# One fused kernel (attention, routed experts, gated convolution): an earlier load of the third pair, and another way through the routing

## The chip, the cores and the metric

The kernel runs on one core of a Trainium2 chip. A core has five engines that run at the same time and wait for each other by semaphores: TensorE (PE, matrix products and transposes), VectorE (DVE), ScalarE (ACT), GpSimd (POOL) and SyncE (SP, which issues transfers). The metric is the device time of one execution in microseconds (us); lower is better.

## The reference, cut to what matters

```python
# attention, per batch (4) and head (8), S = 576 positions, 64 wide
cum = cumsum(max(s, 0)); bias = min(-(cum_i - cum_j), 0)
attn = softmax(causal(q @ k.T / 8 + bias)); x = attn @ v          # x: [4, 576, 512]
# mixture: each token goes to one expert of E = 8
for s in range(S):
    fresh_e = argmax(logits[b, s])
    e = fresh_e if s == 0 or local_gate[b, s] < 0.5 else prev_e   # keeps the last token's expert
    out[b, s] = p[e] * (relu(x[b, s] @ w1[e]) @ w2[e])
# third part: relu(x @ w_in), a convolution of 3 taps along S, sigmoid gate, @ w_out
```

A token whose local gate is 0.5 or more takes the expert of the token before it, so the expert of each token depends on all tokens before it in its batch.

## The kernel before, in words

**Attention** goes over 16 pairs of heads. Each pair's q, k and v come in as natural rows, TensorE turns them (q_nat and k_nat to q_tr and k_tr), and scores are made in nine units per pair. GpSimd makes a bias tile for each unit from ncum_row and ncum_tail, which SyncE loads for each pair from a DRAM copy of the running sums. VectorE adds it to the score (L511), ScalarE takes the exponential, TensorE turns the probabilities (L310) and multiplies with v (L407, L417). The order on each engine is written out by hand; q, k, v and the sums have two buffers each. TensorE multiplies each pair's result with an identity beside the gate weights (L368), so that x and the pair's share of the gate logits come out together; VectorE scales both by the row sums (scale_gates, normalise, and their _end forms for the last tiles). add_heads (L599) sums the eight heads' shares after the last pair of a batch.

**SyncE's queue** is one list (L158 to L191): the sums and q of pair 0, k of pair 1 and sums for pairs 0 and 1; then v of pairs 0 and 1, the gate weights (sync_early, L876 to L880), and then for each pair p: q and k of p + 2, a piece of the first experts' weights, v and sums.

**Routing** follows the last pair. vector_route finds each token's best expert and a code (rank_code: 8 minus its number, or 0 where the token keeps the last expert). Tokens lie in 20 tiles, 5 for each of 4 batches, the fifth with 64 tokens. TensorE turns the codes into 4 rows of 576, one for each batch (L932); VectorE carries the last code that isn't 0 along each row with a scan (L980); TensorE turns the result back (L936). Out of a one-hot table, two matmuls (L940, L941) and some 15 small operations on VectorE come each token's place among rows sorted by expert, the number of 128-row slots of each expert, and by 40 small matmuls (L946) the list of tokens of each of the 25 slots. `then(...)` makes VectorE wait for one operation before the next. The normalising of the last pair, `finish()`, stands between as filler. Behind the token list VectorE makes the numbers that tell TensorE which weights a slot uses (slot_i), the weights of the tokens (mass, picked, chosen, weight) and the columns of the convolution (conv_col).

**Slots.** GpSimd gathers each slot's rows of x (L1047, 25 gathers, two in flight), with two low parts of weights in between. TensorE waits for slot_ready and conv_ready, then for each slot turns x, multiplies with w1 (L1132), turns, and multiplies with w2 (L1145). Weights are split in a high part (ScalarE, L840) and a low part (GpSimd, L850) in a ring of two experts. SyncE loads the second expert's w2 behind the last rows of x (L828, sync_route).

## Time and profile before

| | us |
|---|---|
| median of 3 runs | 791.36 |
| the runs | 791.36, 785.87, 794.63 |
| the profiled execution's time | 788.23 |
| its span | 786.5 |
| TensorE busy | 738.2 (94%) |
| VectorE busy | 427.6 (54%) |
| GpSimd busy | 335.4 (43%) |
| ScalarE busy | 307.8 (39%) |

The span is cut at the first and last instruction, the time includes what lies around it. Attention lasts until about 215 us of the span, the routing until about 237, the slots until about 557, the third part takes the rest. A row of a timeline has start, length, engine, line, operation, output and input, and in brackets how long the engine was idle before it and what released it. Several equal operations in a row are merged (x4), with the length of all.

### The profile page before, as it was taken

How to read it: one execution, taken by the hardware profiler on the slowest of the kernel's cores; microseconds unless marked ns; L12 is line 12 of the kernel's file. 1: busy time of each engine (PE TensorE's matmuls, PEld its weight loads, DVE VectorE, ACT ScalarE, POOL GpSimd, SP SyncE). 2: the span in 40 equal slices, each digit the busy share in tenths (PEclk: the TensorE clock that was granted, in tenths of full speed). 3: DMA queues.
4: the chain of work that ended last, by engine and by line, in shares of the span. 5: the costliest groups of instructions: out<-in, count | busy, mean ns of one | idle time of the engine just before them, and what ended most of it. 6: DMA issues, size and time to landing. Idle time of an engine off the chain costs nothing.

```text
span 786.5 us, 14861 instructions
## 1 busy us (share of the span) xinstructions
PE 738.2 (94%) x4844; PEld 614.8 (78%) x4844; DVE 427.6 (54%) x1022; ACT 307.8 (39%) x608; POOL 335.4 (43%) x439
## 2 busy tenths in 40 slices
PE   6899999999938998999999999999599999999998
PEld 4677877778726886888888888887499998989986
DVE  5577777777684442544435444354259746546420
ACT  4567777777420013111111311100058544535521
POOL 7558787877317449654444764400421100000000
PEclk9999999999958999999999999999789999999999
DMA  8787887864143674334344443200321110000011
GB/s 168 197 214 196 202 212 199 211 178 125 46 135 95 218 226 158 135 130 149 141 166 138 157 154 136 89 28 28 100 63 34 41 48 28 14 36 19 28 41 55
DMA packets 99704, 93.13 MB, mean 118 GB/s; under 512 B 62108, under 2 KB 71604, under 8 KB 99636
## 3 DMA queue, kind: packets, MB, share of 16 engines
q1 hardware_dynamic: 80196, 46.27, 21.9%
q10 hardware_dynamic: 15968, 34.67, 12.6%
q0 software_dynamic: 3472, 11.28, 5.0%
q8 instruction: 44, 0.72, 0.4%
q14 instruction: 24, 0.20, 0.1%
HBM read 76.13 MB, written 16.06 MB: 117 GB/s over the span
## 4 chain that ended last, share of the span: by engine, by line
PE 83%; DMA 6%; POOL 3%; DVE 3%; SPq 2%; issue 2%; ACT 1%; ACTq 0%; POOLq 0%; DVEq 0%
PE row_bank L1145 15%; PE wide_bank L1132 14%; PE wide_bank L1320 13%; PE row_bank L1331 13%; PE score_ps L284 5%; PE turn_ps L407 5%; PE turn_ps L310 5%; DMA x_slots<-x_rows,token_of 5%; PE turn_ps L368 3%; POOL ring L850 2%; PE wide_bank L1156 2%; PE score_ps L278 2%; PE turn_ps L289 2%; PE turn_ps L417 1%; PE bank L1297 1%
## 5 line engine op out<-in xcount | busy, mean ns | idle before, releaser
L850 POOL TENSOR_TENSOR ring<-raw_w,ring 128x2048 fp32r<-128x2048 f32 x30 | 137.6, 4610 | 87.1 <-ACT ring L840 87.0
L1132 PE MATMUL wide_bank<-ring,xs_tr 128*128 x600 | 146.1, 400 | 5.7 <-POOL ring L850 3.2
L1145 PE MATMUL row_bank<-ring,h_tr 128*128 x600 | 143.3, 394 | 1.9 <-DVE h_tr L1203 1.9
L840 ACT ACTIVATE ring<-raw_w 128x2048 fp32r<-128x2048 f32 x30 | 55.8, 1907 | 226.8 <-DMA raw_w<-in_moe_w_dram 197.3
L1132 PEld LDWEIGHTS wide_bank<-ring,xs_tr 128*128 128x128 f32 x600 | 113.1, 192 | 29.5 <-issue 6.6
L1145 PEld LDWEIGHTS row_bank<-ring,h_tr 128*128 128x128 f32 x600 | 110.9, 188 | 24.9 <-issue 2.1
L1320 PE MATMUL wide_bank<-x_tr,ring 128*128 128x288 f32 x768 | 109.8, 301 | 2.5 <-DVE x_tr L1352 2.5
L1320 PEld LDWEIGHTS wide_bank<-x_tr,ring 128*128 128x128 f32 x768 | 105.6, 192 | 3.8 <-DVE x_tr L1352 3.1
L1331 PE MATMUL row_bank<-ring,g_tr 128*128 128x512 f32 x432 | 100.3, 390 | 1.4 <-DVE g_tr L1359 1.4
L1331 PEld LDWEIGHTS row_bank<-ring,g_tr 128*128 128x128 f32 x432 | 80.4, 188 | 17.8 <-DVE g_tr L1359 1.6
L217 POOL TENSOR_SCALAR bias<-ncum_row,cum_col 128x128 f32<-128x128 f32 (+3 forms) x128 | 67.1, 532 | 50.7 <-DVE row_min L511 38.4
L657 ACT ACTIVATE prob<-score,row_min 128x128 f32<-128x128 f32 (+2 forms) x144 | 83.0, 579 | 4.8 <-DVE row_min L511 4.3
L1382 DVE SCALAR_TENSOR_TENSOR conv<-h_pad,conv_col,conv 128x576 f32<-128x576 f32 x64 | 52.3, 817 | 58.4 <-ACT conv L1431 57.2
L511 DVE CUSTOM_DVE_ANT_0 score<-score_ps,bias 128x128 f32<-128x128 f32 (+2 forms) x144 | 71.4, 515 | 9.0 <-PE score_ps L284 4.4
L1189 DVE TENSOR_SCALAR h_sb<-wide_bank 128x512 f32<-128x512 f32 x50 | 34.6, 692 | 71.8 <-PE wide_bank L1132 71.8
L1208 DVE COPY y_sb<-row_bank 128x512 f32<-128x512 f32 x25 | 17.3, 694 | 102.5 <-PE row_bank L1145 102.5
L1277 POOL DMA_INDIRECT y_tok<-y_sorted,place_i x20 | 20.6, 1030 | 106.9 <-PE bank L1297 53.4
L284 PE MATMUL score_ps<-k_tr,q_tr 64*128 64x128 f32 (+3 forms) x256 | 48.8, 481 | 1.6 <-issue 0.9
L310 PE MATMUL turn_ps<-identity,prob 128*128 128x128 f32 x320 | 49.7, 278 | 0.0
L1047 POOL DMA_INDIRECT x_slots<-x_rows,token_of x25 | 23.9, 955 | 54.9 <-DVE token_of L1013 28.4
L407 PEld LDWEIGHTS turn_ps<-prob_tr,v_nat 128*64 128x64 f32 x640 | 34.3, 137 | 14.0 <-issue 13.9
L1422 ACT ACTIVATE h_pad<-wide_bank 128x576 f32<-128x576 f32 x32 | 20.9, 654 | 60.8 <-PE wide_bank L1320 60.7
(180 smaller groups left out, 967.1 us busy)
## 6 DMA issues: line engine op xcount, KB each, us to landing
raw_w<-in_moe_w_dram ACTq DMA_DIRECT2D x12, 2048.0 KB, 9.8
ncum_row<-cum_rows SPq DMA_DIRECT2D x15, 512.0 KB, 4.0
y_sorted<-y_sb SPq DMA_DIRECT2D x25, 256.0 KB, 2.0
raw_w<-in_moe_w_dram SPq DMA_DIRECT2D x12, 512.0 KB, 4.0
ncum_tail<-cum_rows SPq DMA_DIRECT2D x32, 144.0 KB, 4.4
out_dram<-out_sb ACTq DMA_DIRECT2D x18, 256.0 KB, 2.0
v_nat<-in_v_dram SPq DMA_DIRECT2D x32, 128.0 KB, 2.5
q_nat<-in_q_dram SPq DMA_DIRECT2D x30, 128.0 KB, 3.7
```

The lines of the kernel that those rows point to most:

```text
L217: return nc.gpsimd.tensor_scalar(out, row, col, 1.0, ALU.add, ALU.mult)
L284: nc.tensor.matmul(out[:, hh, 0:(i + 1) * P], q_tr[u][at, i * P:(i + 1) * P], k_tr[u][at, 0:(i + 1) * P], start=True, stop=True).then_inc( ...
L310: last = nc.tensor.transpose(bank[:, at + j * P:at + (j + 1) * P], prob[unit(p, n) % 4][:, j * P:(j + 1) * P], identity[:, :])
L407: last = nc.tensor.matmul(bank[at, at_q:at_q + P], v_nat[p % 2][:, j, at], prob_tr[i][:, hh, j * P:(j + 1) * P], start=j == 0, stop=j == i)
L511: nc.vector.tensor_tensor_reduce(out=o, in0=a, in1=b, scale=1.0, scalar=3.0e38, op0=ALU.add, op1=ALU.min, accum_out=row_min[:, at % 4:at % ...
L657: nc.scalar.activation(prob[at % 4][:, 0:w], score[at % 3][:, 0:w], ACT.Exp, bias=row_min[:, at % 4:at % 4 + 1], scale=-1.0, accum_out=row ...
L840: nc.scalar.activation(high, whole, ACT.Copy).then_inc(high_ready, 1)
L850: nc.gpsimd.tensor_tensor(low, whole, high.bitcast(F32), ALU.subtract).then_inc(low_ready, 1)
L1132: last = nc.tensor.matmul(h_bank[:, half, :], xs_tr[:, a, kb, :], ring[:, bass.ds(n, 1), b, at:at + FH].rearrange("p a c -> p (a c)"), sta ...
L1145: last = nc.tensor.matmul(y_bank[:, :], h_tr[:, a, kb, :], ring[:, bass.ds(n, 1), 2 + b, kb * D:(kb + 1) * D].rearrange("p a c -> p (a c)" ...
L1320: last = nc.tensor.matmul(wide_bank[j % 2][:, half, 0:HALF], ring[:, 0, w, col:col + P], x2_tr[:, x, kb, at:at + HALF], start=kb == 0 and ...
L1331: last = nc.tensor.matmul(row_bank[outs % 2][:, :], g_tr[:, a, kb, lo:hi], ring[:, 0, 2 + w, kb * D:(kb + 1) * D], start=kb == 0 and (a, w ...
```

## The change

Three things change.

1. SyncE issues q and k of pair 2 right after the sums of pair 1, in front of v of pairs 0 and 1, with the gate weights between the two v.
2. The routing turns the codes as 20 rows of 128, one for each tile, in one transpose, and scans these. Each tile's last value is spread by a matmul to all partitions; VectorE scans these 20 ends (carry) and gives each token that hasn't found a code in its own tile the carry of the tiles before. Two rounding steps fall away by a larger rounding constant, the constants (back, slot_at, inside, tile_token) are made at the start, and the sum over heads is split: six heads one pair earlier, the last two by additions. The filler is now in two pieces.
3. The weights of the tokens and conv_col move from the routing to behind the first slot's move_x; TensorE waits for conv_ready before the first product with w2 instead of before the first slot.

```diff
         load_cum(1)
+        load_qk(2)
         sp.wait_ge(zeros_ready, 1)
         load_v(0)
+        early(sp)
         load_v(1)
-        early(sp)
         for p in range(PAIRS):
             if p + 2 < PAIRS:
-                load_qk(p + 2)
+                if p:
+                    load_qk(p + 2)
                 between(sp, p)
...
         def add_heads(p):
-            if p % PER_B == PER_B - 1:
-                b = p // PER_B
+            b, at = p // PER_B, slice(p // PER_B * NT, (p // PER_B + 1) * NT)
+            if p % PER_B == PER_B - 2:
                 dve.wait_ge(part_begun, p + 1)
                 dve.wait_ge(part_ready, p + 1)
-                nc.vector.tensor_reduce(logit[:, NT * b:NT * (b + 1), :], gate_part[:, :, :, :].rearrange("p i h e -> p i e h"),
-                                        AX.X, ALU.add).then_inc(logit_ready, 1)
+                nc.vector.tensor_reduce(logit[:, at, :], gate_part[:, :, 0:H - 2, :].rearrange("p i h e -> p i e h"),
+                                        AX.X, ALU.add).then_inc(logit_part, 1)
+            if p % PER_B == PER_B - 1:
...
+                nc.vector.tensor_tensor(logit[:, at, :], logit[:, at, :], gate_part[:, :, H - 2, :], ALU.add).then_inc(logit_part, 1)
+                dve.wait_ge(logit_part, 2 * b + 2)
+                nc.vector.tensor_tensor(logit[:, at, :], logit[:, at, :], gate_part[:, :, H - 1, :], ALU.add).then_inc(logit_ready, 1)
...
         scale_gates_end(PAIRS - 2)
+        add_heads(PAIRS - 2)
         move_tail_end(PAIRS - 1)
...
-    ROUND = 1.5 * 2.0 ** 23
+    ROUND = 1.5 * 2 ** 30
...
     def tensor_route(pe):
...
-        for i in range(TB):
-            n = min(P, S - i * P)
-            last = nc.tensor.transpose(code_rows[:, i * P:i * P + n], by_batch[0:n, i, :], identity[0:n, 0:n])
-        last.then_inc(code_turned, 1)
+        nc.tensor.transpose(wide_bank[0][0:T, 0, 0:P], small["rank_code"][:, :], identity[:, :]).then_inc(code_turned, 1)
         pe.wait_ge(seq_ready, 1)
-        for i in range(TB):
-            last = nc.tensor.transpose(bank[0][:, i * B:(i + 1) * B], expert_seq[:, i * P:(i + 1) * P], identity[0:B, 0:B])
-        last.then_inc(expert_turned, 1)
+        nc.tensor.matmul(bank[0][:, T:2 * T], expert_seq[:, P - 1:P].to_broadcast([T, P]), identity[0:T, 0:T], start=True, stop=True)
+        nc.tensor.transpose(bank[0][:, 0:T], expert_seq[:, :], identity[0:T, 0:T]).then_inc(expert_turned, 1)
...
-        V.memset(expert_seq[:, S:TB * P], 0.0)
-        finish()
+        V.memset(row_is[TAIL:P, :, :].rearrange("p (b i) c -> p b i c", i=TB)[:, :, TB - 1, :], 0.0)
+        V.memset(carry[:, 0:1], 0.0)
...
-        V.tensor_tensor_scan(expert_seq[:, 0:S], keep[:, :], code_rows, 0.0, ALU.mult, ALU.add).then_inc(seq_ready, 1)
+        V.tensor_tensor_scan(expert_seq[:, :], keep[:, :], code_rows, 0.0, ALU.mult, ALU.add).then_inc(seq_ready, 1)
+        finish[0]()
...
+        then(V.tensor_scalar(carry_keep[:, :], ends, 0.0, None, ALU.is_equal))
+        then(V.tensor_tensor_scan(carry[:, 1:1 + T], carry_keep[:, :], ends, 0.0, ALU.mult, ALU.add))
+        then(V.scalar_tensor_tensor(expert[:, :], inner, 0.0, carry[:, 0:T], ALU.is_equal, ALU.mult))
+        then(V.tensor_tensor(expert[:, :], inner, expert[:, :], ALU.add))
...
+        finish[1]()
...
-        V.tensor_tensor(slot_token[:, 0, :, :], slot_is[:, :, :], slots_across(token[:, 0, :]), ALU.mult)
+        V.tensor_scalar(slot_token[:, 0, :, :], slot_is[:, :, :], inside[:, :], None, ALU.mult)
...
         def output(s):
             n = weights_of(s, PIECES // 2)
+            if s == 0:
+                pe.wait_ge(conv_ready, 1)
...
         pe.wait_ge(slot_ready, 1)
-        pe.wait_ge(conv_ready, 1)
         turn_x(0, 0, 0)
...
         move_x(0)
+        vector_weights(dve, then)
         relu(0)
```

On SyncE, at the start, behind the loads of pair 1's sums, the rows before were:

```order
L125 DMA v_nat<-in_v_dram 128x4x64 [waits zeros_ready]
L125 DMA v_nat<-in_v_dram 128x4x64
L126 DMA v_nat<-in_v_dram 64x2x64
L125 DMA v_nat<-in_v_dram 128x4x64 x2
L126 DMA v_nat<-in_v_dram 64x2x64
L876 DMA gates<-in_moe_w_gate_dram 64x4x8 [waits gates_zero]
```

and now they are:

```order
L125 DMA q_nat<-in_q_dram 128x4x64 [waits tails_turned,k_turned]
L125 DMA q_nat<-in_q_dram 128x4x64
L126 DMA q_nat<-in_q_dram 64x2x64
L125 DMA k_nat<-in_k_dram 128x4x64 x2
L126 DMA q_nat<-in_k_dram 64x2x64
L125 DMA v_nat<-in_v_dram 128x4x64 [waits zeros_ready]
L125 DMA v_nat<-in_v_dram 128x4x64
L126 DMA v_nat<-in_v_dram 64x2x64
L896 DMA gates<-in_moe_w_gate_dram 64x4x8 [waits gates_zero]
```

Six issues for q and k of pair 2 (the tail of k lies in q_nat) moved in front, past both v and the gates; pair 1's v now follows the gates.

On VectorE, in the routing, from the codes to the first product's result, before:

```order
L973 TENSOR_TENSOR shifted<-logit,top 128x160
L974 MEMSET expert_seq 4x64
L562 TENSOR_TENSOR x_nat<-turn_ps,row_inv 128x384 [waits x_stored1]
L580 TENSOR_TENSOR x_nat<-turn_ps,row_inv 128x128 [waits tail_end_turned,tails_turned,out_end_turned,inv_part]
L580 TENSOR_TENSOR x_nat<-turn_ps,row_inv 64x128
L979 TENSOR_SCALAR keep<-wide_bank 4x576 [waits code_turned]
L980 SCALAR_TENSOR_TENSOR expert_seq<-keep,wide_bank 4x576 [waits route_step]
L983 TENSOR_TENSOR onehot<-bank,code 128x160 [waits expert_turned]
L989 SCALAR_TENSOR_TENSOR upto<-tile_keep,wide_bank 128x160 [waits ranked]
```

and now (late holds the one-hot table):

```order
L991 MEMSET row_is 64x4x64
L992 MEMSET carry 128x1
L996 TENSOR_SCALAR keep<-wide_bank 20x128 [waits code_turned]
L997 SCALAR_TENSOR_TENSOR expert_seq<-keep,wide_bank 20x128 [waits route_step]
L564 TENSOR_TENSOR x_nat<-turn_ps,row_inv 128x384 [waits x_stored1]
L1002 TENSOR_SCALAR carry_keep<-bank 128x20 [waits expert_turned]
L1003 SCALAR_TENSOR_TENSOR carry<-carry_keep,bank 128x20 [waits route_step]
L1004 SCALAR_TENSOR_TENSOR expert<-bank,carry 128x20 [waits route_step]
L1005 TENSOR_TENSOR expert<-bank,expert 128x20 [waits route_step]
L1006 TENSOR_TENSOR late<-expert,code 128x160 [waits route_step]
L582 TENSOR_TENSOR x_nat<-turn_ps,row_inv 128x128 [waits tail_end_turned,tails_turned,out_end_turned,inv_part]
L582 TENSOR_TENSOR x_nat<-turn_ps,row_inv 64x128
```

The scanned rows went from 576 to 128 wide, four operations on 20 columns came in, and the normalising (x_nat) moved from in front of keep to behind the scan and behind the one-hot table.

## Rows read from the trace of the kernel before

**Rows 1.** The page, part 1: busy time and share of TensorE.

```profile
PE 738.2 (94%) x4844; PEld 614.8 (78%) x4844; DVE 427.6 (54%) x1022; ACT 307.8 (39%) x608; POOL 335.4 (43%) x439
```

**Rows 2.** Timeline of TensorE: start, length, line, operation; in brackets idle before, releaser.

```profile
26.03 0.66 PE L289 MATMUL turn_ps<-identity,q_nat 128*128 128x128 f32 x4 [2.79 <-DMA q_nat<-in_k_dram]
28.52 1.53 PE L407 MATMUL turn_ps<-prob_tr,v_nat 128*64 128x128 f32 x24
...
212.02 0.66 PE L417 MATMUL turn_ps<-tail_tr,v_nat 128*64 128x64 f32 x16
```

**Rows 3.** Timeline of SyncE's queue (issues), and landing times of q_nat's transfers.

```profile
12.50 1.14 SPq L125 DMA_DIRECT2D v_nat<-in_v_dram  x2
...
20.61 0.93 SPq L125 DMA_DIRECT2D q_nat<-in_q_dram  x2
...
24.09 0.59 SPq L889 DMA_DIRECT2D raw_w<-in_moe_w_dram  x1
...
219.58 0.53 SPq L828 DMA_DIRECT2D raw_w<-in_moe_w_dram  x1
...
DMA to landing us min/median/max: 2.4/3.8/5.0
```

**Rows 4.** Groups of TensorE, 30 to 200 us: busy, mean ns, idle before.

```profile
L310 PE MATMUL turn_ps<-identity,prob 128*128 128x128 f32 x278 | 43.2, 278 | 0.0
```

**Rows 5.** Timeline of VectorE through the routing.

```profile
214.83 0.79 DVE L599 TENSOR_REDUCE logit<-gate_part 128x45 f32<-128x360 f32 x1
...
218.38 0.73 DVE L979 TENSOR_SCALAR keep<-wide_bank 4x576 f32<-4x576 f32 x1
219.15 1.34 DVE L980 TENSOR_TENSOR_SCAN expert_seq<-keep,wide_bank 4x576 f32<-4x576 f32 x1
221.28 0.33 DVE L983 TENSOR_TENSOR onehot<-bank,code 128x160 f32<-128x160 f32 x1 [0.78 <-PE bank L936]
222.59 0.49 DVE L989 TENSOR_TENSOR_SCAN upto<-tile_keep,wide_bank 128x160 f32<-128x160 f32 x1 [0.99 <-PE wide_bank L940]
223.12 0.17 DVE L990 TENSOR_SCALAR tiles_of<-upto 128x8 f32<-128x8 f32 x1
...
227.02 0.68 DVE L1008 TENSOR_TENSOR slot_token<-slot_is,token 128x500 bf16<-128x500 bf16 x1
...
228.21 3.34 DVE L1011 TENSOR_SCALAR row_is<-index,row 128x128 bf16<-128x128 bf16 x20
...
236.45 0.18 DVE L1038 COPY conv_col<-row_bank 128x24 f32<-128x24 f32 x1
...
244.31 0.69 DVE L1189 TENSOR_SCALAR h_sb<-wide_bank 128x512 f32<-128x512 f32 x1 [5.03 <-PE wide_bank L1132]
```

**Rows 6.** Timeline of TensorE: the first slot's turning, and the later stall.

```profile
236.74 1.08 PE L1113 MATMUL bank<-identity,x_slots 128*128 128x128 f32 x4 [4.67 <-DVE conv_col L1038]
...
301.87 7.05 PE L1132 MATMUL wide_bank<-ring,xs_tr 128*128 x24 [3.17 <-POOL ring L850]
```

**Rows 7.** Timeline of GpSimd: third gather.

```profile
236.87 0.94 POOL L1047 DMA_INDIRECT x_slots<-x_rows,token_of  x1 [1.47 <-DMA x_slots<-x_rows,token_of]
```

**Rows 8.** Timeline of VectorE at the start.

```profile
8.77 0.29 DVE L492 COPY cum_col<-turn_ps 128x128 f32<-128x128 f32 x1 [1.93 <-PE turn_ps L254]
...
9.91 0.69 DVE L538 COPY k_tr<-turn_ps 128x512 f32<-128x512 f32 x1 [0.57 <-PE turn_ps L289]
...
34.85 0.29 DVE L511 CUSTOM_DVE_ANT_0 score<-score_ps,bias 128x128 f32<-128x128 f32 x1 [0.20 <-PE score_ps L284]
```

**Rows 9.** Timeline of GpSimd: the biases of pair 2.

```profile
32.34 0.72 POOL L217 TENSOR_SCALAR bias<-ncum_row,cum_col 128x128 f32<-128x128 f32 x2 [6.14 <-DMA ncum_tail<-cum_rows]
```

**Rows 10.** The gathers (L1047), 230 to 300 us.

```profile
DMA to landing us min/median/max: 3.2/3.6/9.2
```

**Rows 11.** Transfers of raw_w, 210 to 305 us.

```profile
DMA to landing us min/median/max: 7.8/10.1/14.3
```

**Rows 12.** Windows: length, busy time of PE, PEld, DVE, ACT, POOL, PEclk, DMA, GB/s.

```profile
301.80:304.00 2.20, 2.13 (x5) 1.75 (x6) 0.00 (x0) 1.82 (x2) 2.10 (x1) 0.50 0.82 255
```

More of the change, by code:

```diff
@@ L787, in mixture @@
     x_slots = sb("x_slots", [P, SLOTS, D], where=region)
+    late = sb("late", [P, D], where=region)
+    exps = late[:, 0:T * E].rearrange("p (t e) -> p t e", e=E)
+    oh, picked = (late[:, n * T * E:(n + 1) * T * E].rearrange("p (e t) -> p e t", e=E) for n in (1, 2))
+    mass = late[:, 3 * T * E:3 * T * E + T]
     route = ExitStack()
-    small = {n: sb(n, [P, T], where=route) for n in ("top", "flag", "rank_code", "mass", "chosen", "place", "slot", "row")}
-    by_token = {n: sb(n, [P, T, E], where=route) for n in ("is_top", "shifted", "exps")}
-    by_expert = {n: sb(n, [P, E, T], where=route) for n in ("onehot", "upto", "where_to", "picked")}
+    small = {n: sb(n, [P, T], where=route) for n in ("top", "flag", "rank_code", "place", "slot", "row")}
+    by_token = {n: sb(n, [P, T, E], where=route) for n in ("is_top", "shifted")}
+    by_expert = {n: sb(n, [P, E, T], where=route) for n in ("upto", "where_to")}
     per_e = {n: sb(n, [P, E], where=route) for n in ("tiles_of", "tiles_upto", "base")}
-    keep = sb("keep", [B, S], where=route)
-    expert_seq = sb("expert_seq", [B, TB * P], where=route)
+    keep = sb("keep", [T, P], where=route)
+    expert_seq = sb("expert_seq", [T, P], where=route)
+    carry_keep, expert = (sb(n, [P, T], where=route) for n in ("carry_keep", "expert"))
+    carry = sb("carry", [P, 1 + T], where=route)
     slot_is = sb("slot_is", [P, T, SLOTS], BF16, where=route)
```

105 lines of the change are left out of this document (56 added, 49 removed).

## The prediction

> **What bounds the kernel now.** I read the page first: TensorE is busy 94% of the span [rows 1], so a gain must take idle time away from it, or from the chain where it has nothing to do. The timelines, engine by engine, show the places and price them; three matter.
>
> *The start.* TensorE stands idle 2.79 us before it turns pair 2's q, and what ends the wait is the last piece of q_nat to land [rows 2]. SyncE's queue shows why: v of two pairs from 12.50 us, the gates behind them, and pair 2's q only from 20.61 [rows 3]. After this TensorE never waits until the last pair: its commonest group between 30 and 200 us has 0.0 idle before it [rows 4], and so have the other eleven there. So what is won at the start moves the whole attention part.
>
> *The routing.* From 214.83 us (sum of the gate products) VectorE works down one chain, with TensorE between, to the 20 row_is comparisons at 228.21 us [rows 5]. Nothing else can run, and the first slot's turning begins at 236.74 us [rows 6].
>
> *The slots.* From there TensorE is nearly full, with one stall of 3.17 us before 301.87 us, ended by GpSimd's low parts of the third expert [rows 6], which stand in its queue behind the 25 gathers.
>
> **Part 1: the load order.** The six q and k issues take the places that the first v had. From 12.50 us, six issues take about 3.5 us (from 20.61 to the weight piece at 24.09 now, six of the same sizes), so the last is issued by 16.0 us and, at the longest landing of 5.0 us [rows 3], in by 21. Their new wait, for pair 0's k and tails to be turned, was over at 10 us (VectorE copies the turned k at 9.91 [rows 8]), so nothing queues behind it. TensorE is free for the turning at 26.03 - 2.79 = 23.24 us. The stall goes whole: **2.79 us**. What is queued behind: v of pair 0 is issued by about 18 us and in by 23, wanted at 28.52 - 2.79 = 25.73 us [rows 2]; gates are wanted some 7 us later still; v of pair 1 by 38 us. The total of SyncE's issues before 24.09 us is the same, so everything from the first weight piece on keeps its time.
>
> What is late next is pair 2's row of sums. GpSimd begins its biases at 32.34 us, 6.14 us idle before, released by ncum_tail [rows 9], which is issued behind the weight piece of 24.09 and isn't moved. Two additions (0.72) and half of the masks (0.54) later, about 33.3, the first is ready. VectorE takes it at 34.85 today, waiting only 0.20 for TensorE [rows 8]; 2.79 earlier would be 32.06. So VectorE gets a new wait of 1.3 us. Behind it stand scaling and normalising pair 0, moving the last prob tile of pair 1, and pair 2's next scores. TensorE asks for those two scores before its third product, at about 37.1 us now, 34.3 then; they are done at 33.3 + 0.5 = 33.8. The wait is absorbed, with 0.5 us to spare. If it were not, 1.5 us of the 2.79 would remain. I take 2.79, and keep 1.5 for the range; above it nothing, for no more idle time is there.
>
> GpSimd's extra iotas (two more than before, under half a microsecond each if they are like its 128-column bias additions, 0.72 for two [rows 9]) and VectorE's five small copies in place of four operations come before cum_col at 8.77 us, where VectorE has stood 1.93 us idle [rows 8]: zero.
>
> **Part 2: the routing, step by step** [rows 5], positive is saved:
> - logit: a reduction of 0.79 us becomes two additions of 45 columns. The nearest row, 0.17 us for 8 columns plus 0.02 to 0.04 between dependent operations, gives 0.40 for both: +0.4. The six-head reduction stands earlier, ahead of copying tail_end_tr at 210.90; at 270 of 360 columns it takes about 0.6, and the product that needs the copy comes after 212.02 [rows 2]: 211.2 + 0.6 = 211.8, covered by 0.2. Without that cover it costs up to 0.4.
> - the first turning: rank_code is out at 217.35, keep starts at 218.38, with normalising (0.49 and 0.46) in between. Now one transpose of 128 columns instead of five (five took 0.75), beside shifted and two memsets (256 columns and one; at keep's 1.0 ns a column 0.3). Keep starts some 0.75 instead of 1.2 us after rank_code begins: +0.4, bounds 0 and 0.6.
> - keep 576 to 128 wide: 0.73 against 0.17 for 8 gives 1.0 ns a column, so 0.29: +0.44.
> - scan: 1.34 for 576, 0.49 for 160 columns; 128 give 0.42: +0.92.
> - turning back: 0.78 idle with five small matmuls 0.11 apart; with two, 0.45 to 0.5, and normalise (0.49) fits in it: +0.28.
> - the carry: four more dependent operations on 20 columns, 0.18 + 0.02 each: -0.82.
> - normalise_end goes behind onehot, under the 0.99 us in which VectorE waits for ranked: zero.
> - one rounding step less for tiles_of and one for slot, 0.2 each: +0.41; row without a wait behind it: +0.1.
> - the first slot_token, 500 columns, becomes a tensor_scalar on bf16. Bounds: 0.68 today, and 0.17 apart for row_is (3.34 for 20), the same operation at 128 columns. I take 0.38, nearer the row that is the same operation: +0.3, bounds 0 and 0.5.
> The Trainium skill, page "VectorE: DVE Perf Modes", section "The perf-mode tier table", says that tensor_scalar on 16-bit data in SBUF may run at four elements a cycle and tensor_tensor at two; by it the 500 columns would be an estimated 0.26 us and the sum 0.12 better. The trace does not agree for the second of the two: a tensor_tensor of 500 bf16 columns takes 0.68 us [rows 5], about what keep's 1.0 ns a column gives with one element a cycle, so I don't lean on it for the first.
>
> Sum: 0.4 + 0.4 + 0.44 + 0.92 + 0.28 - 0.82 + 0.41 + 0.1 + 0.3 = **2.4 us**, between 1.4 (the two open terms and the turning back at nothing) and 2.8 (the two at their upper ends).
>
> **Part 3: weights behind the first slot's move.** Today conv_col ends at 236.63 [rows 5] and the turning starts at 236.74 [rows 6]. But gather 2, which waits for gather 0 to land, starts at 236.87 [rows 7], so the slot's data landed no later than that and probably just before. Both waits end together, so taking one away gives next to nothing. I take zero; it matters only in that VectorE's 2.2 us can't become the bound. In their new place they lie in VectorE's 5.03 us idle before relu(0) [rows 5].
>
> SyncE's load of the second expert's w2 waits behind the last x rows. It was issued at 219.58 [rows 3]; x rows now end some 1.8 us later in the routing, 221.4 on today's scale, while the first gather, today about 3.9 us before the third, so at 233.0, moves to 230.6. Weight loads took 7.8 us to landing at best [rows 11], and nothing else loads here: 229 to 230, just clear.
>
> **Sum.** 2.79 + 2.4 = 5.2 us. The profiled execution took 788.23 (span 786.5), so it would be 783.0. It lies 3.1 below the median of the three runs; the four executions average 789.9, and I predict from these: **784.7 us**.
>
> **Rivals.**
> 1. *The sums take over from q and k.* VectorE's new wait of 1.3 us does reach TensorE. For it: only 0.5 us to spare. Against: TensorE works through banks two deep. Gain 3.9: 786.0. Chance 0.15.
> 2. *The routing isn't shorter.* The added dependent steps and normalise, now inside the chain, eat it; gain 2.8 or less: 787. For: every short step costs 0.2 whatever its width. Against: the two 576-wide rows alone lose 1.36. Chance 0.1.
> 3. *Slower: w2's load runs into the first gathers.* Place: GpSimd's first four gathers, two in flight. Gathers land after 3.6 us at the median, 9.2 at the longest [rows 10], in the stretch with weight loads; such a load took up to 14.3 us to landing [rows 11]. It decides if the load takes over 9.2 us here. At 14.3 it lies beside both pairs of gathers; half of 9.2 - 3.6 for each pair is 2.8. TensorE starts 2.8 later, GpSimd is behind by 2.8 more, and the stall before 301.87 grows by that: 5.6 us against 5.2 won, 790.3. A clock that falls longer than today (0.50 granted, the 1.2 GHz level, just after that stall [rows 12]) would come on top. For: the load is hardly clear. Against: nothing else loads then. Chance 0.06.
> 4. *The stall at 301.87 goes as well.* Gathers get ahead of TensorE by 3 us; then another 4.3 us (3.17, and 1.1 for the 2.2 us at half clock [rows 12]): 780.4. Against: gathers and TensorE both start from gather 0, and the load that slows the gathers is tied to TensorE. Chance 0.07.
> The forecast keeps 0.62.
>
> **Range and chances.** The four executions spread by 8.8 us, a median less: 3 us either way. With gains from 2.8 to 6 around that, 779 to 790 leaves out less than 2 in 10. One per cent, 7.9 us, is about what a measurement of this kernel can tell from no change. The forecast is 0.7%, so most cases stay within it; rival 4 and the lucky side of the forecast pass it: faster 0.3, same 0.65, slower 0.05.
>
> **What would show it.** Right: no idle row before pair 2's q, GpSimd's biases for pair 2 still at about 32.3 and VectorE's first score of pair 2 waiting for them; gate sum to row_is 11.0 us instead of 13.4; first turning released by the gather; 3 us stall unchanged. Wrong: TensorE idle near 34 or 25 us, a first gather over 4 us, another length of the stall, or the first turning less than 4 us earlier than 236.74.

## The result and the profile after

| | before | after |
|---|---|---|
| median of 20 runs each, us | 790.82 | 783.88 |
| lowest and highest | 784.57, 796.98 | 778.56, 790.53 |
| ratio of the times, 95% interval | | 0.9916 [0.9894, 0.9938] |
| the profiled execution's time | 788.23 | 785.70 |
| its span | 786.5 | 784.0 |

The change gains 6.6 us, give or take 1.7; 784.7 was predicted. The ratio leaves out executions that took over 1.5% more than the fastest of their kernel, so it gives 6.6 us where the medians of all 20 differ by 6.9. The two profiled executions lie only 2.5 us apart in span. So the work is to find what the change gives in every execution, and what in some.

The page, part 1, answers to [rows 1]; VectorE was at 427.6 us before:

```profile
PE 739.0 (94%) x4838; PEld 614.9 (78%) x4838; DVE 436.3 (56%) x1034; ACT 308.0 (39%) x608; POOL 335.0 (43%) x442
```

**The start.** Timeline of TensorE of the kernel after (columns as in [rows 2]):

```profile
23.07 0.66 PE L357 MATMUL turn_ps<-identity,prob 128*128 128x128 f32 x4
23.56 0.60 PE L291 MATMUL turn_ps<-identity,q_nat 128*128 128x128 f32 x4
...
25.99 1.20 PE L409 MATMUL turn_ps<-prob_tr,v_nat 128*64 128x128 f32 x18
```

No bracket stands before pair 2's q where 2.79 us stood [rows 2]. The first product with v starts at 25.99 us and not 28.52: 2.53 earlier. This trace had come to the stretch later than the one before, as the same scores show, before and after:

```profile
19.86 0.49 PE L284 MATMUL score_ps<-k_tr,q_tr 64*128 64x128 f32 x4 [0.86 <-issue]
...
20.34 0.49 PE L286 MATMUL score_ps<-k_tr,q_tr 64*128 64x128 f32 x4 [0.86 <-issue]
```

From these scores to the first product with v it is 8.66 us before and 5.65 after, 3.01 less. GpSimd and VectorE at pair 2's sums:

```profile
32.58 0.72 POOL L219 TENSOR_SCALAR bias<-ncum_row,cum_col 128x128 f32<-128x128 f32 x2 [5.90 <-DMA ncum_tail<-cum_rows]
```

```profile
33.58 0.29 DVE L513 CUSTOM_DVE_ANT_0 score<-score_ps,bias 128x128 f32<-128x128 f32 x1 [1.46 <-POOL bias L236]
...
36.60 0.56 DVE L513 CUSTOM_DVE_ANT_0 score<-score_ps,bias 128x384 f32<-128x384 f32 x1 [0.61 <-POOL bias L236]
```

The sums come at 32.58 us (32.34 before, [rows 9]) and VectorE waits 1.46 us for them, where 1.3 was forecast. TensorE's timeline has no idle time there.

**The attention.** The products with v of one pair start 12.39 us after those of the pair ahead, before the change, in all pairs but the last two. After it, the pair in which a batch's sum over heads is finished takes 12.70 to 12.72, three times: 0.95 us in all, which nobody forecast. VectorE, groups between 60 and 200 us (busy, mean ns, idle), and then its timeline and GpSimd's in the first of the three pairs:

```profile
L609 DVE TENSOR_TENSOR logit<-logit,gate_part 128x45 f32<-128x45 f32 x3 | 3.6, 1195 | 0.1
L607 DVE TENSOR_TENSOR logit<-logit,gate_part 128x45 f32<-128x45 f32 x3 | 3.0, 1004 | 0.0
```

```profile
75.86 1.07 DVE L607 TENSOR_TENSOR logit<-logit,gate_part 128x45 f32<-128x45 f32 x1
76.97 1.20 DVE L609 TENSOR_TENSOR logit<-logit,gate_part 128x45 f32<-128x45 f32 x1
```

```profile
75.59 2.50 POOL L883 TENSOR_TENSOR ring<-raw_w,ring 128x512 fp32r<-128x512 f32 x2
```

The two additions of 45 columns take 1.07 and 1.20 us. GpSimd's two subtractions of 512 columns (half of the 2.50 us each) end at 76.84 and 78.09; the additions end at 76.93 and 78.17, right behind each. In the third batch the first addition takes 0.88. After the last batch, with GpSimd idle, the same two take 0.21 and 0.20 us.

**The routing.** VectorE's timeline, the rows that answer to [rows 5]:

```profile
213.24 0.21 DVE L607 TENSOR_TENSOR logit<-logit,gate_part 128x45 f32<-128x45 f32 x1
213.48 0.20 DVE L609 TENSOR_TENSOR logit<-logit,gate_part 128x45 f32<-128x45 f32 x1
...
215.31 0.18 DVE L989 TENSOR_TENSOR rank_code<-rank_code,flag 128x20 f32<-128x20 f32 x1
...
216.13 0.27 DVE L996 TENSOR_SCALAR keep<-wide_bank 20x128 f32<-20x128 f32 x1
...
216.44 0.41 DVE L997 TENSOR_TENSOR_SCAN expert_seq<-keep,wide_bank 20x128 f32<-20x128 f32 x1
216.78 0.52 DVE L564 TENSOR_TENSOR x_nat<-turn_ps,row_inv 128x384 f32<-128x384 f32 x1
217.66 0.18 DVE L1002 TENSOR_SCALAR carry_keep<-bank 128x20 f32<-128x20 f32 x1 [0.36 <-PE bank L953]
...
219.85 0.49 DVE L1012 TENSOR_TENSOR_SCAN upto<-tile_keep,wide_bank 128x160 f32<-128x160 f32 x1 [0.60 <-PE wide_bank L956]
...
223.74 0.35 DVE L1027 TENSOR_SCALAR slot_token<-slot_is,inside 128x500 bf16<-128x500 bf16 x1
...
224.60 3.33 DVE L1032 TENSOR_SCALAR row_is<-back,row 128x128 bf16<-128x128 bf16 x20
```

From the sum of the gates to row_is it is 224.60 - 213.24 = 11.36 us, against 228.21 - 214.83 = 13.38 [rows 5]: 2.02 saved, 2.4 forecast. To the first turning of x it is 2.12.

**The first slot.** TensorE, ScalarE, GpSimd and VectorE of the kernel after:

```profile
233.03 1.09 PE L1136 MATMUL bank<-identity,x_slots 128*128 128x128 f32 x4 [4.59 <-DMA x_slots<-x_rows,token_of]
235.83 8.04 PE L1155 MATMUL wide_bank<-ring,xs_tr 128*128 x24 [1.71 <-DVE xs_tr L1207]
```

```profile
229.46 3.71 ACT L860 ACTIVATE ring<-raw_w 128x2048 fp32r<-128x2048 f32 x2 [13.36 <-DMA raw_w<-in_moe_w_dram]
```

```profile
235.48 4.56 POOL L870 TENSOR_TENSOR ring<-raw_w,ring 128x2048 fp32r<-128x2048 f32 x1
```

```profile
235.49 0.31 DVE L1058 TENSOR_REDUCE late<-late 128x20 f32<-128x160 f32 x1
235.84 4.24 DVE L1059 TENSOR_SCALAR late<-late 128x20 f32<-128x20 f32 x1
240.11 0.28 DVE L1060 RECIPROCAL late<-late 128x20 f32<-128x20 f32 x1
```

The turning starts at 233.03 us, 3.71 earlier than 236.74 [rows 6], released by its gather and no longer by conv_col. The load of w2 has landed at 229.46; GpSimd's issue of the first gather starts at 229.36 and takes 1.17 us, so the two hardly meet. New and unforeseen is the second of the moved weights: a tensor_scalar on 20 columns, 4.24 us long, ends 0.04 us behind GpSimd's subtraction of 2048 columns. The reduction ahead of it ran beside the same subtraction in 0.31 us. Behind the turning the first slot takes longer than before: the second slot's turning follows after 10.68 us (at 243.71) and not 10.13 (at 246.87 before), and the third slot's starts 3.15 us earlier than before (251.74 against 254.89), not 3.71. Windows over the first slot, before and after, show why:

```profile
236.74:246.87 10.13, 8.42 (x29) 0.68 0.31 92
...
233.03:243.71 10.68, 8.97 (x29) 0.64 0.35 98
```

As 2 x (1 - PEclk) x length, this is 6.5 us at clock 0.50 before and 7.7 after. The slot that starts earlier has more of its work at the lower level, which gives back some 0.6 us.

**The stall near 300 us**, and windows of TensorE (length, PE busy, PEclk, DMA share, GB/s):

```profile
299.30 5.96 PE L1155 MATMUL wide_bank<-ring,xs_tr 128*128 x19 [3.83 <-POOL ring L870]
```

```profile
300.00:302.00 2.00, 2.00 (x6) 0.50 1.02 418
```

The stall is 3.83 us after, 3.17 before [rows 6], both followed by a stretch at clock 0.50 (1.2 GHz).

### The profile page after: what moved, and what is told of

Same layout as the page of the kernel before. It is cut to its first block, busy times and chain, and to the rows that moved or that the text cites. A ratio compares the mean times of both kernels' runs of the same rounds, so it can differ in the third digit from the quotient of the medians.

```text
span 784.0 us, 14869 instructions
## 1 busy us (share of the span) xinstructions
PE 739.0 (94%) x4838; PEld 614.9 (78%) x4838; DVE 436.3 (56%) x1034; ACT 308.0 (39%) x608; POOL 335.0 (43%) x442
## 4 chain that ended last, share of the span: by engine, by line
PE 59%; DMA 5%; POOL 3%; DVE 2%; issue 2%; ACT 1%; ACTq 0%; POOLq 0%; SPq 0%; DVEq 0%
PE row_bank L1170 15%; PE wide_bank L1155 14%; PE row_bank L1356 13%; PE wide_bank L1345 12%; DMA x_slots<-x_rows,token_of 5%; POOL ring L870 2%; PE wide_bank L1181 2%; PE bank L1322 1%; PE bank L1136 1%; POOL x_slots L1070 1%; DMA y_tok<-y_sorted,place_i 0%; PE bank L962 0%; DVE x_tr L1377 0%; DMA y_sorted<-y_sb 0%; ACT x_tr L1429 0%
## 5 line engine op out<-in xcount | busy, mean ns | idle before, releaser
L1170 PE MATMUL row_bank<-ring,h_tr 128*128 x600 | 144.9, 397 | 1.9 <-DVE h_tr L1227 1.9
L1447 ACT ACTIVATE h_pad<-wide_bank 128x576 f32<-128x576 f32 x32 | 20.9, 653 | 59.6 <-PE wide_bank L1345 59.4
```

The lines of the kernel that those rows point to most:

```text
L1170: last = nc.tensor.matmul(y_bank[:, :], h_tr[:, a, kb, :], ring[:, bass.ds(n, 1), 2 + b, kb * D:(kb + 1) * D].rearrange("p a c -> p (a c)" ...
```

## Experiments

Two theories stood. **Account A:** the change is worth what its rows show, 2.5 (start) - 0.95 (heads) + 2.1 (routing up to the first turning), and what lies above that is chance at the stall near 300 us and in the clock. **Account B:** all of the 6.6 us belongs to the change. Beside it there was one question on the long VectorE operations: do they wait for GpSimd's whole instruction?

| run | median, us | before, same call | ratio, 95% interval |
|---|---|---|---|
| 1 order alone | 788.87 | 790.53 | 0.9971 [0.9931, 1.0011] |
| 2 all but the order | 789.75 | 790.53 | 0.9981 [0.9949, 1.0013] |
| 3 heads whole | 780.89 | 790.53 | 0.9872 [0.9827, 0.9916] |
| 4 weights ahead | 785.75 | 790.53 | 0.9911 [0.9878, 0.9945] |
| 5 low parts between gathers | 778.94 | 789.94 | 0.9865 [0.9825, 0.9906] |
| 6 edits 3, 4 and 5 together | 778.25 | 789.94 | 0.9855 [0.9817, 0.9894] |
| 9 before + edit 5 | 786.10 | 791.80 | 0.9940 [0.9916, 0.9963] |
| 10 order alone + edit 5 | 782.41 | 791.80 | 0.9889 [0.9855, 0.9922] |
| 11 all but the order + edit 5 | 783.89 | 791.80 | 0.9924 [0.9887, 0.9960] |
| 12 the change + edit 5 (as 5) | 779.79 | 791.80 | 0.9861 [0.9828, 0.9895] |

**1. The order alone**, on the kernel before:

```diff
+        load_qk(2)
         sp.wait_ge(zeros_ready, 1)
         load_v(0)
-        load_v(1)
         early(sp)
+        load_v(1)
...
-                load_qk(p + 2)
+                if p:
+                    load_qk(p + 2)
```

> The kernel before with the new order of the first loads alone; routing, the sum of heads and the place of the weights stay as before. My account: the idle time of 2.79 us in front of the third pair's q goes, TensorE's first pv starts near 25.99 us instead of 28.52 (2.5 us earlier), all pairs keep the period of 12.39 us, and the first turning starts at about 234.2 instead of 236.74. Time 788.3, about 2.5 us under the kernel before. Rival A (the loads move the whole loss of 0.95 us into the attention, by queue time): pairs of 12.7 us appear here too, and the first turning starts at about 235.2. Rival B (later waits take the start's gain back): the first turning stays at 236.7 and the time at 790.8.

No idle time before pair 2's q; the first product with v at 26.29 us; every pair but the shorter last two takes 12.39 or 12.40; first turning at 234.79, where 234.2 was expected. So the order does not stretch the pairs: rival A falls, and so does rival B, by which the turning stays at 236.7. The trace's span is 780.9, lower than the changed kernel's own, though its turning is later: the stall near 300 us was short:

```profile
297.45 5.72 PE L1134 MATMUL wide_bank<-ring,xs_tr 128*128 x24 [0.61 <-POOL ring L852]
```

The later expectations count it as 0; it is 0.61 us, with no stretch at clock 0.50 behind it. The median of the same runs is 788.87. The traced execution took 782.67, 6 us less.

**2. All but the order:** the changed kernel with the reverse of that diff.

> The changed kernel with the old order of the first loads. My account: the idle time of 2.8 us in front of the third pair's q is back, three pairs still take 12.7 us and not 12.39, since that comes from the additions of the heads' sum, and the first turning starts at 233.03 + 2.5 = 235.5 us. The time is that of the kernel before less 6.6 us plus 2.5: about 786.7, a gain of 4.1 for the rest of the change. If the two halves don't add up, this run and the one with the order alone will miss 6.6 us in their sum: a sum under 5 would say that part of the gain is luck of the clock or of the interval.

The idle time is back (2.31 us), and three pairs take 12.70 to 12.72. But the time came out 3 us above the forecast and the first turning at 238.45, also 3 us later than forecast; and the two halves give 2.3 + 1.5 = 3.8 us where the whole gives 6.6, each with an interval of 3. The trace shows what the expectation had left out. TensorE behind the idle time:

```profile
25.90 1.11 PE L289 MATMUL turn_ps<-identity,q_nat 128*128 128x128 f32 x4 [2.31 <-DMA q_nat<-in_k_dram]
...
28.39 2.08 PE L284 MATMUL score_ps<-k_tr,q_tr 64*128 64x512 f32 x4
30.40 2.56 PE L407 MATMUL turn_ps<-prob_tr,v_nat 128*64 128x128 f32 x24
```

```profile
24.00:60.00 36.00, 34.10 (x303) 0.91 0.78 199
```

The four scores take 2.08 us where 1.13 is usual, and the mean clock of 24 to 60 us is 0.91: 2 x (1 - 0.91) x 36 = 6.5 us at clock 0.50. From the turning of q to the first product with v it is 4.50 us, against 2.49 before, and the next pair's products follow after 13.42 and not 12.39: 3.0 us lost. The idle time of the start can cost more than its own length.

**3. The heads' sum whole for the first three batches**, on the changed kernel:

```diff
-            if p % PER_B == PER_B - 2:
+            split = b == B - 1
+            if split and p % PER_B == PER_B - 2:
...
+            if not split and p % PER_B == PER_B - 1:
...
+                nc.vector.tensor_reduce(logit[:, at, :], gate_part[:, :, :, :].rearrange("p i h e -> p i e h"),
+                                        AX.X, ALU.add).then_inc(logit_ready, 1)
```

> The changed kernel, but the sum over the heads is one reduction for batches 0 to 2, as before the change, and is split only for the last batch, whose sum the routing waits for. Theory 1 (a VectorE operation with two inputs in SBUF stands still while GpSimd works on an operation of the same kind): the two additions of 1.07 and 1.20 us in three pairs are gone, one reduction of 0.8 us stands in their place, all pairs take 12.39 us, the first turning starts 0.95 us earlier than in the changed kernel (232.1), and the time is 0.9 us less. Theory 2 (the new order of loads is what stretches the three pairs): they still take 12.7 us and the time is the same.

Same place as the two additions above:

```profile
76.72 0.81 DVE L607 TENSOR_REDUCE logit<-gate_part 128x45 f32<-128x360 f32 x1
```

It runs in 0.81 us beside GpSimd's subtractions of 76.45 to 78.97 us, no pair takes over 12.40, and from pair 0's products with v to pair 14's it is 172.96 us instead of 173.91: the 0.95 us are back. Theory 1 holds, theory 2 falls. In absolute time the turning stayed at 233.03, since this execution had started 0.86 us slower (first product with v at 26.85). The median of 780.89 is 3 us under the changed kernel's, more than 0.95; with six runs that is within the interval.

**4. The weights back ahead of the first slot's move:**

```diff
-        move_x(0)
         vector_weights(dve, then)
+        move_x(0)
```

> The changed kernel with the weights of VectorE put back ahead of the first slot's move, as before the change. Theory 1 (the same rule as for the heads): the tensor_scalar at the start of the late weights, 4.24 us in the changed kernel beside GpSimd's subtraction of 128x2048, takes 0.2 us again, and the eviction of the first hidden (relu) ends some us earlier; but the weights' row operations run in front of the first turning's eviction only if they lie in VectorE's way before the gather lands. The first gather lands near 233.0 and the weights' start is at about 228.5, so they are done before it: the time is the same or up to 0.3 us less, since the first output waits for the second product over the hidden slots and not for relu alone. Theory 2 (the move of the weights was itself worth something): 0.5 to 1 us more than the changed kernel.

```profile
233.54 0.30 DVE L1058 TENSOR_REDUCE late<-late 128x20 f32<-128x160 f32 x1
233.87 0.18 DVE L1059 TENSOR_SCALAR late<-late 128x20 f32<-128x20 f32 x1
```

0.18 us instead of 4.24, and the turning (235.77) still waits for its gather alone. The time, 785.75, can't be told from the changed kernel. From the first maximum of the logits to the turning it is 235.77 - 216.51 = 19.26 us, and 19.24 in the changed kernel: part 3 of the change, and taking it back, are both worth nothing there. Behind the turning this first slot takes 10.29 us and not 10.68, at a mean clock of 0.66 and not 0.64; by the same sum as above that is 7.0 us at clock 0.50 and not 7.7, worth 0.35 of the 0.39. So nothing is left for the weights behind the turning either. The 2.7 us by which this trace is later arose at the start, where matmuls still ran at double length until 20.9 us.

**7. picked first among the weights**, on the changed kernel:

```diff
+        then(V.tensor_tensor(picked[:, :, :], oh[:, :, :], exps[:, :, :].rearrange("p t e -> p e t"), ALU.mult))
         then(V.tensor_reduce(mass[:, :], exps[:, :, :], AX.X, ALU.add))
...
-        then(V.tensor_tensor(picked[:, :, :], oh[:, :, :], exps[:, :, :].rearrange("p t e -> p e t"), ALU.mult))
```

> The changed kernel with the multiplication of picked (two inputs in SBUF) as the first instruction of VectorE's late weights. In the changed kernel the first one, a reduction with one input, took 0.31 us, and the second, a tensor_scalar on 128x20, 4.24 us beside GpSimd's subtraction of 128x2048, where it takes 0.2 us elsewhere. Theory 1a (an operation of VectorE that needs what GpSimd holds waits for GpSimd's whole instruction, and two inputs in SBUF are one such need): picked takes some 4 us, and the tensor_scalar 0.18, as GpSimd's instruction is over by then or the next one costs it again. Theory 1b (it is that line's own affair, such as an input written by the reduction just ahead): picked takes 0.45 and the tensor_scalar 4 us again.

```profile
235.84 4.81 DVE L1058 TENSOR_TENSOR late<-late 128x160 f32<-128x160 f32 x1
240.69 0.32 DVE L1059 TENSOR_REDUCE late<-late 128x20 f32<-128x160 f32 x1
241.04 0.18 DVE L1060 TENSOR_SCALAR late<-late 128x20 f32<-128x20 f32 x1
```

GpSimd's subtraction runs from 235.76 to 240.32 here. picked, 0.45 us elsewhere, now takes the 4.81, and the tensor_scalar 0.18: theory 1a. It is not the line but what runs beside it. Three forms were seen to wait: additions of 45 columns (0.9 to 1.2 us beside 512 columns of GpSimd), a product of 160 columns (4.81 beside 2048) and a tensor_scalar of 20 columns (4.24 beside 2048). Reductions were seen not to (0.31 and 0.81 us).

The Trainium skill has this rule, on the page "SBUF — State Buffer", section "Who interferes with whom": VectorE's second pair of ports is GpSimd's only one, and whoever issues first holds it for the whole instruction. VectorE needs it for a second SBUF input, against a GpSimd operation that reads SBUF, and for copies and tensor_scalar in the modes that use two ports, never for a reduction on this chip. The traces agree for the additions, the tensor_scalar, picked and the reductions: GpSimd had started 0.27 us ahead of the first addition, 0.13 ahead of the second, 0.36 ahead of the tensor_scalar and 0.08 ahead of picked. The rule was there to be read, and the prediction priced the additions without it. The time was 780.24 us, span 778.3, with a stall of 0.39 near 300 us: the 4 us that VectorE loses are no loss of time. Of its next work, relu(0), it does the first half at 242.34 and then waits 1.63 us for TensorE, whose row of products runs on without idle time from 236.18. This is one execution.

**8. The changed kernel once more.**

> The changed kernel once more, for a second trace of it. Expected: the shares of the account repeat to 0.1 us where no gather or clock is in them (three pairs of 12.7 us, from the first maximum of the logits at 213.8 to the first turning 19.2 us), and three places differ from trace to trace: how early in the start the matmuls run at full speed (up to 2.7 us on the first pv), the wait for the low part near 300 us (2.7 to 5.4), and the clock behind it.

This too is one execution. Three pairs of 12.70 to 12.72 again, and from the first maximum to the turning 232.82 - 213.52 = 19.30 us (19.24 in the first trace). Span 780.4, 3.6 less than its first trace: first product with v 0.27 earlier, the stall 1.80 instead of 3.83.

**5. Two low parts in front of the last five gathers**, on the changed kernel:

```diff
-        gather_slots(pool, 8, SLOTS)
-        with pool.Fori(1, E // 2) as i:
+        gather_slots(pool, 8, 20)
+        low_part(pool, 2, 0, 0)
+        low_part(pool, 2, 0, 1)
+        gather_slots(pool, 20, SLOTS)
+        low_part(pool, 2, 0, 2)
+        low_part(pool, 2, 0, 3)
+        low_parts(pool, 3, 1)
+        with pool.Fori(2, E // 2) as i:
```

> The changed kernel with two of GpSimd's low parts of the third expert pair's weights put in front of the last five gathers, and not behind all of them. In six traces so far TensorE waited 3.2, 3.8, 0, 5.4, 5.0 and 2.7 us for that low part near 300 us, and ran at clock 0.50 for some 3 to 4 us behind the longer of these waits. My account: the wait is gone (under 0.5 us) and no stretch at 0.50 near 300 us is left, the turning that followed the one at 288.50 after 17.74 us follows it after 12.3 to 13; time 779 to 781, 3 to 5.5 us under the changed kernel, and fewer runs far from the fastest. Rival: the last gathers, now later, are wanted by TensorE before they land, or the low part waits for ScalarE's high part; then a wait of 2 us or more stands elsewhere and the time is that of the changed kernel within 1 us.

GpSimd and TensorE of this kernel:

```profile
277.47 9.17 POOL L870 TENSOR_TENSOR ring<-raw_w,ring 128x2048 fp32r<-128x2048 f32 x2
286.80 0.96 POOL L1070 DMA_INDIRECT x_slots<-x_rows,token_of  x1 [0.16 <-issue]
```

```profile
295.30 5.71 PE L1161 MATMUL wide_bank<-ring,xs_tr 128*128 x24
300.85 0.60 PE L1142 MATMUL bank<-identity,x_slots 128*128 128x128 f32 x4
```

The stall is gone and so is the stretch at 0.50; the turning follows the one at 288.58 after 12.27 us. Median 778.94, 4.9 us under the changed kernel (4.0 if each is set against the kernel before of its own call). The rival falls: the last gather, some 9 us later, is not missed.

**6. Edits 3, 4 and 5 together.**

> The changed kernel with three edits together: the heads' sum split for the last batch alone, VectorE's weights ahead of the first slot's move, and the two low parts in front of the last five gathers. If the edits add up: 0.95 us for the heads, 0 to 0.3 for the weights, 3 to 5.5 for the low parts, so 4 to 6.5 us under the changed kernel, 777 to 780, and 10 to 13 us under the kernel before. If the low parts bring nothing: 782 to 783.

778.25 us, the fastest kernel of this study, 11.7 us under the one before in its call. No pair over 12.40, turning at 231.59, no stall, span 775.8. It lies 0.7 us under number 5, where 0.95 was due; such a difference is too small for these runs, but the trace has it.

**9 to 12. The change and its halves, without the stall.** Edit 5 was put into four kernels, run in one call: before, the order alone, all but the order, the whole change.

> The kernel before with two low parts in front of the last five gathers, so without the wait near 300 us that differs from run to run (0 to 5.4 us in seven traces). Beside the next three kernels, which have the same edit, it shows the change and its halves without that wait. My account: the change is worth 2.5 (start) less 0.95 (heads) plus 2.1 (routing) plus 0.25 (18 slots at 12.266 and not 12.280 us), so 3.9 us, and this kernel takes 778.9 + 3.9 = 782.8. Rival (the 6.6 us measured are the change's own worth, not luck at 300 us): 785.5.

> As the kernel just ahead, with the new order of the first loads besides: 2.5 us less, 780.3; if the start's idle time also costs a stretch at clock 0.50 behind it in part of the runs (as in the trace of the changed kernel with the old order, where the second pv came 13.42 us after the first and not 12.39), up to 2 us more than that.

> The change without the new order of the loads, with the two low parts in front of the last five gathers: by the routing and the heads alone 2.1 + 0.25 - 0.95 = 1.4 us less than the kernel before with the low parts, 781.4, the idle time of 2.8 us in front of the third pair's q back.

> The whole change with the two low parts in front of the last five gathers, the same kernel as was measured at 778.94, now in one call with the three others. Expected 778.9. The two halves add up if this one lies as far under the kernel with the low parts alone as the two halves together: 2.5 + 1.4 = 3.9 us.

Medians: 786.10, 782.41, 783.89, 779.79. The order gives 3.7 us without the rest and 4.1 with it, the rest 2.2 and 2.6, together 5.9 against 6.3 for the whole: the halves add up. The whole is 0.9940 - 0.9861 = 0.0079 of the time, with an uncertainty of about 0.0040, or 3 us. None of the four traces has a stall near 300 us. Account A's 782.8 for the kernel before is missed, account B's 785.5 is nearer, and the stall is out of all four; but with 3 us of uncertainty this run alone does not rule out A's 3.9. The main measurement does, as its interval starts at 4.9. So what lies above 3.9 us is probably not the stall. The clock tells more. Time at clock 0.50, as 2 x (1 - PEclk) x length of a window, in us (PEclk has two digits, so a value is good to 0.4 us in the shortest window and to 1 us in the longest; in brackets the stall):

| trace | 24 to 60 | 205 to 250 | 250 to 330 (stall) | 500 to 600 | span |
|---|---|---|---|---|---|
| before | 0 | 24.3 | 3.2 (3.17) | 18.0 | 786.5 |
| 9 | 0 | 27.0 | 0 | 14.0 | 780.5 |
| 2 | 6.5 | 24.3 | 6.4 (5.4) | 18.0 | 790.3 |
| 11 | 3.6 | 24.3 | 0 | 14.0 | 781.9 |
| 1 | 0 | 27.0 | 0 (0.61) | 18.0 | 780.9 |
| 10 | 0 | 24.3 | 0 | 20.0 | 780.2 |
| after | 0 | 24.3 | 3.2 (3.83) | 18.0 | 784.0 |
| 8 | 0 | 24.3 | 3.2 (1.80) | 14.0 | 780.4 |
| 7 | 0 | 24.3 | 0 (0.39) | 14.0 | 778.3 |
| 3 | 0 | 24.3 | 6.4 (5.0) | 18.0 | 785.2 |
| 4 | 0 | 24.3 | 3.2 (2.7) | 18.0 | 785.5 |
| 5 | 0 | 24.3 | 0 | 14.0 | 777.0 |
| 12 | 0 | 24.3 | 0 | 14.0 | 778.0 |
| 6 | 0 | 24.3 | 0 | 14.0 | 775.8 |

The first four rows are the kernels that keep the idle time of the start. In two of these four the clock fell behind it, for 6.5 and 3.6 us; in the ten others never. At half the clock a busy stretch loses half its length, so this is worth up to 3.3 and 1.8 us in those executions (3.0 and 1.5 by the rows from q's turning on). Rows of number 11 and number 9 for the same window:

```profile
24.00:60.00 36.00, 33.47 (x311) 0.95 0.80 206
```

```profile
24.00:60.00 36.00, 34.31 (x353) 1.00 0.82 216
```

All runs have a mean clock, and those of number 11 fall in two groups: five at 0.974 to 0.976 took 781.28 to 783.89 us, four at 0.965 to 0.967 took 786.57 to 788.02. Of the twelve runs of the same kernel with the new order (5 and 12), eleven lie at 0.972 to 0.976 and one at 0.969. This fits a clock that falls behind the start's idle time in part of the executions, though only the traces say where it fell. So the clock is the likely reason why the order is worth 3.7 to 4.1 us and not the 2.5 of the rows; four traces don't fix how often it comes, and number 9's is of its fastest run (782.26, median 786.10).

The medians of the mean clock are 0.969 (9), 0.970 (10), 0.974 (11) and 0.9755 (12). Most of the rise goes with the rest of the change, not with the order. The mean also counts stretches in which TensorE is idle, so it is no measure of time lost. The table shows one such difference: around the routing, the clock stood at 0.50 for 27 us in two of the four traces with the old routing (9 and 1) and for 24 in the two others and in all ten with the new. That lies mostly in the routing's idle time; how much of the rest's gain it is stays open. The last but one column shows why single spans mislead: 20.0 us in number 10 and 14.0 in number 9 are an estimated 3 us of time at most, and they hide the 2.51 us by which number 10 was ahead at the first product with v.

Number 12 shows something else. Its sums for pair 2 came 1.2 us later than in the trace after:

```profile
33.81 0.72 POOL L219 TENSOR_SCALAR bias<-ncum_row,cum_col 128x128 f32<-128x128 f32 x2 [6.62 <-DMA ncum_tail<-cum_rows]
```

```profile
35.42 0.92 PE L286 MATMUL score_ps<-k_tr,q_tr 64*128 64x384 f32 x4 [0.32 <-DVE row_min L513]
```

TensorE waited, and from the first pair's products with v to the second's it took 12.99 us instead of 12.39. This is rival 1 at nearly half of its price of 1.3. TensorE itself was 0.49 us later than in the trace after, so the sums were 0.74 late against it and cost 0.60: about 0.1 us was to spare, not the 0.5 of the prediction.

## Why the prediction was right, point by point

- **The start, 2.79.** Right. The first product with v is 2.53 earlier, and 3.01 from the same scores on, as the trace after had begun 0.48 later. The idle time that goes is 2.16 to 2.79 us from trace to trace, and numbers 9 and 10 differ by 28.18 - 25.67 = 2.51. The six issues took some 4.6 us and not 3.5 (12.87 to 17.5), which did no harm. Missing in the sum was what stands behind an idle stretch: in two of four traces the clock fell. The order is worth 3.7 to 4.1 in the medians.
- **The new wait of VectorE.** 1.46 us for 1.3; absorbed in nearly every trace, as said, and once not (0.60 us in number 12). The place was right in forecast and rival, but the margin was nearer to 0.1 us than to 0.5. That it held in the trace after was close.
- **The sum of the heads.** This is the step that failed. It was priced at +0.4 in the routing, "covered" for the early part, and the additions of the three other batches were not priced at all, as they were thought to cost 0.2 each anywhere. They cost 0.9 to 1.2 beside GpSimd, and 0.95 us of the path. In the routing the step gave 0.27: from the start of the sum to the first maximum it is 213.79 - 213.24 = 0.55 us, and 0.82 before. The net is a loss, and experiment 3 takes it back.
- **The rest of the routing, 2.4 with the heads.** 2.02 to row_is, 2.1 to the turning. Against the terms: scan 1.34 to 0.41 (0.93, forecast 0.92), keep 0.73 to 0.27 (0.46, forecast 0.44), first slot_token 0.68 to 0.35 (0.33, forecast 0.3), first turning: from rank_code's start to keep 0.82 us, forecast 0.75. The steps from upto to the first slot_token gave 0.54 (4.43 to 3.89 us, forecast 0.51), and the carry cost 0.87 (forecast 0.82). Mis-sized was the turning back: 0.28 was forecast and nothing came. normalise was said to fit in the wait; it starts as the scan ends and fills 0.52 us, and VectorE then still waits 0.36 for TensorE, so from the scan's end to carry_keep it is 0.81 us, and it was 0.79 to onehot before. normalise_end behind the one-hot table cost nothing, as forecast: from the table's start to upto's it is 1.31 us before and 1.32 after.
- **The weights' move, zero.** Right, by experiment 4 (19.26 and 19.24 us). And for the stated reason, both waits ending together: with the weights ahead the turning waits for its gather alone. That the weights would fit in VectorE's 5.03 us of idle time was only just so: with the wait for GpSimd they took 6.3 us (235.49 to 241.79) and not 2.2.
- **The load of w2.** Landed at 229.46; forecast 229 to 230, "just clear". The first gather was issued at 229.36 and not 230.6, so it was not clear in the way that was meant, and rival 3 did not come even so.
- **The stall unchanged at 3 us.** Wrong as a statement on the kernel. In the eight traces with the old order of gathers it was 0.39, 0.61, 1.80, 2.7, 3.17, 3.83, 5.0 and 5.4 us, whatever the rest of the kernel. Rival 4 was put down as something that the change might do with a chance of 0.07; it is a draw that both kernels make in each execution, and its length goes with how long the gathers take. The spread of the runs is 12.0 us in the changed kernel (20 runs) and 4.6 with edit 5 (two times six), and nothing here shows that the draw favours one of the two.
- **The total.** 5.2 were forecast, from a mean of four executions of 789.9 that should read 790.0. The steady rows give 2.5 - 0.95 + 2.1 = 3.7 at the first turning, less some 0.6 for the first slot's clock, and 0.25 more from slots of 12.266 us instead of 12.280 (18 of them), whose reason was not looked for. The prediction named as a sign of being wrong a first turning less than 4 us earlier than 236.74, and another length of the stall; both came (3.71 us, and 3.83 for 3.17). The medians give 6.3 and 6.6, so some 3 us, with an uncertainty as large, are not in the steady rows; the clock behind the start's idle time is a seen part of it. The forecast came out close because one loss that was missed and one gain that was missed nearly cancel, and that is luck.

## What to carry to other kernels

Before a short two-input operation of VectorE is added or moved, look at what GpSimd runs at that time: its price here was not its own row, but what was left of GpSimd's instruction. An idle stretch of TensorE is priced with what the clock may do behind it; and where gathers stand in an in-order queue ahead of a part that TensorE wants, the part goes in between them. When a profile's difference and the difference of the medians disagree, take the same measurement again with the variable stall taken out of both kernels.

## What the runs showed of the hardware

- A VectorE operation with two inputs in SBUF, and a tensor_scalar of 20 f32 columns, lasted until GpSimd's two-input subtraction ended: 4.24 and 4.81 us beside 2048 columns, 0.9 to 1.2 beside 512, against 0.18 to 0.45 with GpSimd idle or gathering. Its own width shows only in how far behind GpSimd's instruction it ended: 0.04 us for 20 columns, 0.08 and 0.09 for 45, 0.33 for 160. Reductions beside the same subtractions took 0.31 and 0.81 us.
- At which level TensorE's clock stood behind the same idle time was not the same in each execution: behind the 2.2 to 2.8 us at the start it stayed at 1.00 in two traces and stood at 0.50 for 3.6 and 6.5 us in two others. Behind the stall near 300 us, 0.39 and 0.61 us of idle time came with none, 1.80 us with 3.2 us at 0.50, and 5.0 us with 6.4.
- From the issue of the first gather to the start of the low part behind the last one, GpSimd took 57.1, 57.7, 58.7, 59.2, 59.7, 60.7, 61.3 and 61.4 us in eight traces, and the stalls were 0.61, 0.39, 1.80, 2.7, 3.17, 3.83, 5.0 and 5.4 us: but for the first two, in the same order. GpSimd's idle rows between the gathers are waits for earlier gathers to land.
- A tensor_tensor of 500 bf16 columns with a broadcast input took 0.67 us, a tensor_scalar of the same columns 0.35. By the Trainium skill, page "VectorE: DVE Perf Modes", section "The perf-mode tier table", an estimated 0.26 us was due for the second (four elements a cycle, on top of the fixed part of row_is's 0.17 us for 128 columns); the trace gives 0.09 more. The product that the prediction set against the table's tensor_tensor has such a broadcast input too; no run here has it without one.
